# Feed-forward layers in five token tiles of 464 instead of six of 384

## The reference

```python
# attention with a bias that a small network makes from log distances
x = (log1p(|i-j|) / log1p(max(i,1)))[..., None]
bias = relu(x @ w1 + b1) @ w2                      # one value per head, i, j
attn = softmax(q @ k.T / 8 + bias);  x = attn @ v  # (2304, 512)
# first feed-forward layer ("cosine layer"), 512 -> 2048 -> 512
h = x @ w_in;  x = (h * cos(h)) @ w_out
# second ("gated layer"), 512 -> 1536 -> 512, after an RMS norm
xn = x / sqrt(mean(x*x) + 1e-6) * rms_g
out = (silu(xn @ w_gate) * (xn @ w_val)) @ w_out
```

## Time and profile before

| | |
|---|---|
| median of 3 runs | 1193.43 us (1193.26 to 1194.7) |
| profiled execution | 1196.07 us, span 1194.3 us |
| matmuls in all | 7464, of which 3 x 1632 = 4896 in the two layers |
| cosine layer, a tile | about 67.6 us |
| gated layer, a tile | about 75.0 us |

### The profile page before, as it was taken

The page is one execution under the profiler, slowest core; times in us unless marked ns, Lnnn a source line. Parts: engine busy times, 40 slices in busy tenths (PEclk is TensorE's granted clock), DMA queues, the critical chain, the costliest instruction groups (busy, mean ns, idle before and its releaser), DMA issues.

```text
span 1194.3 us, 21751 instructions
## 1 busy us (share of the span) xinstructions
PE 1164.8 (98%) x7464; PEld 1081.5 (91%) x7464; DVE 661.0 (55%) x1554; ACT 492.9 (41%) x1032; POOL 479.1 (40%) x506
## 2 busy tenths in 40 slices
PE   5879999999999999999999999999999999999998
PEld 2367777777799999999999999999999999999998
DVE  7968888888889857566575786652020020200201
ACT  7867787787833433333333333111111111111211
POOL 0057777777775433424252353851111111111111
PEclk9989999999999999999999999999999999999999
DMA  6844435352134000000000010430000000000000
GB/s 196 261 155 129 160 103 169 101 190 77 62 109 130 19 1 1 0 0 0 0 0 0 0 46 25 132 90 28 1 1 26 0 26 0 0 26 0 26 0 27
DMA packets 46680, 69.10 MB, mean 58 GB/s; under 512 B 3856, under 2 KB 27568, under 8 KB 46640
## 3 DMA queue, kind: packets, MB, share of 16 engines
q1 hardware_dynamic: 46640, 68.61, 18.5%
HBM read 53.26 MB, written 15.34 MB: 57 GB/s over the span
## 4 chain that ended last, share of the span: by engine, by line
PE 61%; issue 28%; POOL 5%; DMA 2%; ACT 2%; DVE 1%; SPq 0%; ACTq 0%; POOLq 0%; DVEq 0%
PE banks L533 7%; PE banks L859 7%; PE banks L861 7%; PE banks L860 7%; PE bank L859 6%; PE bank L861 6%; PE bank L860 6%; PE bank L575 6%; PE bank L559 5%; POOL product_low L1471 5%; PE bank L581 2%; DMA bias_scratch<-bias_stage 1%; PE bias_ps L273 1%; ACT bias_stage L191 1%; PE bank L555 1%
## 5 line engine op out<-in xcount | busy, mean ns | idle before, releaser
L859 PE MATMUL banks<-x_high,w_high_rest 128*128 128x384 f32 x672 | 225.3, 335 | 0.0
L861 PE MATMUL banks<-x_high,w_low_rest 128*128 128x384 f32 x672 | 224.5, 334 | 0.0
L860 PE MATMUL banks<-x_low,w_high_rest 128*128 128x384 f32 x672 | 224.5, 334 | 0.0
L1471 POOL TENSOR_TENSOR product_low<-X,product_high 128x384 fp32r<-128x384 f32 x72 | 72.9, 1013 | 345.2 <-ACT product_high L1414 345.2
L1452 DVE TENSOR_TENSOR X<-X,banks 128x384 f32<-128x384 f32 x72 | 39.8, 552 | 298.6 <-PE banks L861 298.6
L1254 POOL TENSOR_TENSOR product_low<-g,product_high 128x384 fp32r<-128x384 f32 x96 | 103.7, 1081 | 221.5 <-ACT product_high L1127 221.3
L859 PE MATMUL bank<-product_high,w_high_rest 128*128 128x384 f32 x480 | 160.6, 335 | 0.4 <-POOL product_low L1254 0.4
L861 PE MATMUL bank<-product_high,w_low_rest 128*128 128x384 f32 x480 | 160.4, 334 | 0.0
L860 PE MATMUL bank<-product_low,w_high_rest 128*128 128x384 f32 x480 | 160.3, 334 | 0.0
L680 DVE CUSTOM_DVE_ANT_0 probs<-banks,bias 128x576 f32<-128x576 f32 (+1 forms) x160 | 119.7, 748 | 19.5 <-PE banks L533 11.3
L628 ACT ACTIVATE probs<-probs,by_row 128x576 f32<-128x576 f32 (+1 forms) x160 | 123.3, 771 | 9.3 <-DVE by_row L680 8.3
(11 more groups left out here) (118 smaller groups left out, 2518.8 us busy)
## 6 DMA issues: line engine op xcount, KB each, us to landing
raw_qk<-in_qk SPq DMA_DIRECT2D x32, 576.0 KB, 3.8
bias_scratch<-bias_stage SPq DMA_DIRECT2D x36, 288.0 KB, 3.1
bias<-bias_scratch SPq DMA_DIRECT2D x32, 288.0 KB, 3.5
w_raw<-in_w_out SPq DMA_DIRECT2D x28, 256.0 KB, 2.6
values<-in_v SPq DMA_DIRECT2D x16, 320.0 KB, 4.1
w_raw<-in_w_in SPq DMA_DIRECT2D x16, 256.0 KB, 2.8
out_t<-X SPq DMA_DIRECT2D x5, 768.0 KB, 3.5
w_raw<-in_w_gate SPq DMA_DIRECT2D x12, 256.0 KB, 3.1
```

What stands on the lines that cost most here:

```text
L859: nc.tensor.matmul(out, high, x_high, start=start, stop=False)
L860: nc.tensor.matmul(out, high, x_low, start=False, stop=False)
L861: return nc.tensor.matmul(out, low, x_high, start=False, stop=stop)
L1471: pool.tensor_tensor(sl[f % 2][:, :], s, sh[f % 2][:, :].bitcast(F32), ALU.subtract).then_inc(s_split, 1)
```

## The change

The tile width `NT` becomes 464, so 2304 tokens are four tiles of 464 and one of 448 (`NT_LAST`). Every function of the layers takes the width as an argument, and the last tile is written out behind the loop on TensorE as well. The norm works on four pieces of 116 (or 112) tokens. So that the wider buffers fit, `turns`, `angle` and `g` become slices of the buffer that q and k land in, the high and low parts of a product share one buffer, the table of the bias stage lies in `X`, the norm's few words lie in `small`, and `ident` is freed after the cosine layer. In the gated layer the place of a stored tile in `X` is given by a list, and the low part of the last weight unit is made two chunks later.

```diff
-NT = 384
-TILES_T = TOK // NT
+NT = 464
+TILES_T = -(-TOK // NT)
+NT_LAST = TOK - (TILES_T - 1) * NT
...
-SUB = P
-NSUB = NT // SUB
+NSUB = 4
+SUB = NT // NSUB
...
+def widths_of(tile):
+    return tuple(NT if t < TILES_T - 1 else NT_LAST for t in (tile - 1, tile, tile + 1))
...
-    table = sb(ctx, "log_table", [P, LT], F32)
+    table = att.X[:, 0:LT]
...
-        self.ident = sb(top, "ident", [P, P], F32)
+        self.ident = sb(top, "ident", [P, P], F32, "right")
-        self.raw_qk = [sb(ctx, f"raw_qk{h}", [P, 2, S], F32) for h in range(2)]
+        self.raw_both = sb(top, "raw_qk", [P, 4 * S], F32, "right")
+        self.raw_qk = [self.raw_both[:, h * 2 * S:(h + 1) * 2 * S].rearrange("p (i s) -> p i s", i=2) for h in range(2)]
...
-            last = self.nc.tensor.transpose(self.rms_ps[:, i * SUB:(i + 1) * SUB],
-                                            self.inv_rms[:, i:i + 1].broadcast_to([SUB, P]), self.ident[:, :])
+            last = self.nc.tensor.transpose(self.rms_ps[:, i * sub:(i + 1) * sub],
+                                            self.inv_rms[0:sub, i:i + 1].broadcast_to([sub, P]), self.ident[0:sub, 0:sub])
...
+    def add_product(self, sb, ctx, i):
+        both = sb(ctx, f"product{i}", [P, 2, NT], F32R)
+        self.high.append(both[:, 0, :])
+        self.low.append(both[:, 1, :])
...
-        self.turns = sb(ctx, "turns", [P, NT], I32, "right")
-        self.angle = sb(ctx, "angle", [P, NT], F32, "right")
-        self.g = sb(ctx, "g", [P, NT], F32, "right")
+        turns, self.angle, self.g = (room[:, i * NT:(i + 1) * NT] for i in range(3))
+        self.turns = turns.bitcast(I32)
...
-            last = three_products(self.nc, out[:, 0:NT], self.weights, w, k, self.features.xh[:, k, :],
-                                  self.features.xl[:, k, :], k == 0, k == KC - 1)
+            last = three_products(self.nc, out[:, 0:n], self.weights, w, k, self.features.xh[:, k, 0:n],
+                                  self.features.xl[:, k, 0:n], k == 0, k == KC - 1)
...
-        tile(0, True)
-        with pe.Fori(1, T) as t:
-            tile(t, False)
+        tile(0, True, widths_of(0))
+        with pe.Fori(1, T - 1) as t:
+            tile(t, False, widths_of(1))
+        tile(T - 1, False, widths_of(T - 1))
...
+    homes = [min(t + 1, T - 2) for t in range(T - 1)] + [T - 1]
...
                     elif f == 11:
                         for d in range(KC):
-                            norm.scale(dve, T - 1, d)
+                            norm.scale(dve, T - 1, d, NT_LAST)
+                        weights.split_low(dve, LAST_UNIT)
...
                     for w in units(f):
-                        weights.split_low(dve, w)
+                        if w < LAST_UNIT:
+                            weights.split_low(dve, w)
```

More of the change, by code:

```diff
@@ L1072, in _, with up @@
     def _(pe):
-        def up(t, f, first):
+        def up(t, f, first, n):
             if first:
@@ L1077, in up, with down @@
                 pe.wait_ge(g_ready, t * C1 + (f + 1 - h_back[f]))
-            chunks.up(pe, h_ps[h_at[f]], 2 * f, t, f == 0).then_inc(h_ready, 1)
-        def down(t, f, first):
+            chunks.up(pe, h_ps[h_at[f]], 2 * f, t, f == 0, n).then_inc(h_ready, 1)
+        def down(t, f, first, n):
             if first:
@@ L1135, in free_of, with tile @@
             return (down_done, t * DOWNS) if f == 0 else (x1_ready, t * KC)
-        def tile(t, first, last):
+        def tile(t, first, last, widths):
+            back, n, ahead = widths
             for f in range(C1):
                 if not (first and f == 0):
-                    chunks.count_turns(act, h_ps[h_at[f]], t, f)
+                    chunks.count_turns(act, h_ps[h_at[f]], t, f, n)
                 if f == C1 - 1:
@@ L1191, in product, with tile @@
                 dve.wait_ge(g_split, t * C1 + f)
-            dve.tensor_tensor(g[:, :], angle[:, :], h_ps[h_at[f]][:, 0:NT], ALU.mult).then_inc(g_ready, 1)
-        def tile(t, first, last):
+            dve.tensor_tensor(g[:, 0:n], angle[:, 0:n], h_ps[h_at[f]][:, 0:n], ALU.mult).then_inc(g_ready, 1)
+        def tile(t, first, last, widths):
+            back, n, ahead = widths
             for f in range(C1):
@@ L1220, in tile @@
                     att.keep_mixed(dve, PAIRS - 1, 1, att.mixed_end)
[L1221 removed]
+                    product(t, f, first, n)
                 units = first_units(f) if first else [next_unit(f)] if last and next_unit(f) is not None else []
@@ L1345, in _, with up @@
     def _(pe):
-        def up(t, f, which, first):
+        def up(t, f, which, first, n):
             if first:
@@ L1352, in up, with down @@
                 pe.wait_ge(s_ready, t * C2 + (f - 1))
-            chunks.up(pe, val_ps[f % 2] if which else gate_ps, U1 + 3 * f + which, T + t, f == 0 and which == 0
-                      ).then_inc(val_ready if which else gate_ready, 1)
-        def down(t, f, first):
+            chunks.up(pe, val_ps[f % 2] if which else gate_ps, U1 + 3 * f + which, T + t, f == 0 and which == 0,
+                      n).then_inc(val_ready if which else gate_ready, 1)
+        def down(t, f, first, n):
             if first:
@@ L1371, in down, with tile @@
                 last.then_inc(down_done, 1)
-        def tile(t, first):
+        def tile(t, first, widths):
+            back, n, _ = widths
             for f in range(C2):
                 if f >= LAG2:
-                    down(t, f - LAG2, first)
+                    down(t, f - LAG2, first, n)
                 elif not first:
-                    down(t - 1, C2 - LAG2 + f, False)
+                    down(t - 1, C2 - LAG2 + f, False, back)
                 if not (first and f == 0):
-                    up(t, f, 0, first)
-                    up(t, f, 1, first)
+                    up(t, f, 0, first, n)
+                    up(t, f, 1, first, n)
                 if first and f == 6:
-                    norm.means(pe, T - 1)
+                    norm.means(pe, T - 1, NT_LAST)
                 elif first and f == 10:
-                    norm.spread(pe, T - 1)
-        tile(0, True)
-        with pe.Fori(1, T) as t:
-            tile(t, False)
+                    norm.spread(pe, T - 1, NT_LAST)
+        tile(0, True, widths_of(0))
+        with pe.Fori(1, T - 1) as t:
+            tile(t, False, widths_of(1))
+        tile(T - 1, False, widths_of(T - 1))
         for f in range(C2 - LAG2, C2):
-            down(T - 1, f, False)
+            down(T - 1, f, False, NT_LAST)
     @block.scalar
     def _(act):
-        def tile(t, first, last):
+        def tile(t, first, last, widths):
+            _, n, ahead = widths
             for f in range(C2):
@@ L1477, in tile @@
                         if 0 <= i < norm.SQUARE_STEPS:
-                            norm.square_step(pool, T - 1, i)
+                            norm.square_step(pool, T - 1, i, NT_LAST)
                     if f == 7:
-                        norm.power(pool, T - 1)
-        tile(0, True)
-        with pool.Fori(1, T) as t:
-            tile(t, False)
+                        norm.power(pool, T - 1, NT_LAST)
+        tile(0, True, NT)
+        with pool.Fori(1, T - 1) as t:
+            tile(t, False, NT)
+        tile(T - 1, False, NT_LAST)
     ctx.close()
@@ L1522, in build @@
         chunks.add_buffers(sb, top)
-        norm = Norm(nc, sb, sem_of, top, ins, X, banks, rms_ps, att.ident)
+        norm = Norm(nc, sem_of, ins, X, banks, rms_ps, att.ident, small[:, 2:])
         cos_layer_phase(nc, block, sb, sem_of, norm, features, weights, chunks, att)
```

302 lines of the change are left out of this document (158 added, 144 removed).

## The result

| kernel | median us (lowest to highest, executions) | against before, 95% interval |
|---|---|---|
| before | 1194.07 (1192.93 to 1195.12, 6) | 1 |
| after | 1198.30 (1197.58 to 1200.42, 6) | 1.0036 [1.0026, 1.0046] |
| after, measured again | 1197.91 (1196.84 to 1198.96, 10) | 1.0027 [1.0017, 1.0036] |

A forecast was written before the change was run, and what follows sets the result against it. The layers were taken to be bound by TensorE's list of matmuls. Terms of -10.9 for fewer matmuls, +0.4 for the norm and +0.1 for the end summed to -10.4 us, giving a median of 1183.0 us, range 1181.0 to 1188.0.

The forecast's parts named there:

- Fewer, wider matmuls: In the layers, 4080 matmuls instead of 4896, same columns streamed; 816 times a fixed 13.3 ns excess saved, 10.9 us.
- Grows with width: Rival: each layer matmul's excess over its columns grows with width, so the gain vanishes; 1193.9 us, chance 0.06.
- Addresses: Rival: 1760 layer matmuls whose moving rows start 64 bytes off run slower; at 13.3 ns each 1206.4 us, chance 0.07.
- New waits: Rival: DVE's splitting no longer fits behind 12 matmuls at eight tile starts, costing 3.0 us; 1186.0 us, chance 0.09.
- The norm: Means and spread on four pieces: 1.27 us a tile, 6.4 for five tiles against 6.0 for six; cost 0.4 us.
- The tile starts: Waits where tiles begin: helpers grow less than the down matmuls covering them; no change, bounds -0.5 and +0.5 us.
- the chains inside a chunk: DVE, ACT and POOL work within chunks of both layers stays covered by TensorE's matmuls; cost nothing.
- the moved low weight part: One 0.68 us DVE instruction behind four scalings, before gated tile 1: nothing, at most 0.7 us.
- attention's end: DVE and ACT split the wider first cosine tile there, some 0.6 us more beside other work; nothing, at most 0.6.
- Shared buffers and code: Shared buffers change addresses, not instructions, and the written-out last tile runs without gaps: nothing, unless addresses count.
- The program's end: Last of four copies and last store after TensorE, with 64 more columns: about 0.1 us more.
- The cosine layer's first tile: 338 matmuls take 69.9 us; some 62 DVE instructions widen by about 75 ns, DVE busy 59.3 us, 85% instead of 93%.

The follow-up runs named there:

- e2: The changed kernel with tiles still 464 but rows of `x_high`, `x_low` and `product` 480 long, all starts at multiples of 128 bytes: 1194.26 us, 0.9996 of before.
- e1: The changed kernel with `NT` back at 384, so six tiles, keeping the shared buffers and written-out last tile: 1193.92 us, 0.9996 of before.
- e5: The changed kernel with four tiles of 512 and one of 256, rows of `x_high`, `x_low` and products 512 long: 1190.01 us, 0.9957 of before.
- e6: The changed kernel with four tiles of 496 and one of 320, on rows 512 long: 1197.02 us, 1.0015 of before.
- e7: e5 with the norm's steps in the short last cosine tile one or two chunks later: 1189.03 us, 0.9949 of before.

## Why the prediction was wrong

*The step that failed* is "Fewer, wider matmuls". It took the excess over the columns as 13.3 ns for any width. At 464 it is 17.1 and at 448 it is 16.2 ns. Against the forecast this makes 3264 x (210.4 - 206.7) + 816 x (202.9 - 200.0) = 12.1 + 2.4 = 14.5 us. 816 matmuls less were to bring 10.9. In terms of the sum: the excess was 4896 x 13.6 = 66.6 us and is 3264 x 17.1 + 816 x 16.2 = 69.0, so +2.4 stands where -10.9 stood. (The 1.2 us between 14.5 - 10.9 and 2.4 are the base: starts of 384 columns lie 173.6 ns apart over all 4860, not 173.3.) With 0.2 for the norm and 0.55 less idle time, +2.4 makes 2.05 us; the layers grew by 1.9. Of the 3.8 ns that 464 columns have over 13.3, 1.0 goes with the row length, by e2, and 2.8 stay with the width; a lone burst shows 3.3.

*Why the evidence did not carry.* The argument went from two widths, 384 and 288, to a third. The reading itself was right: 133.1 ns is the mean of 311 such distances in attention. But the two widths proved nothing about a third: in bursts 320, 352, 384, 400 and 512 share 13.3 ns, and 416 to 480 do not; and a burst of 288 has 131.8, an excess of 11.8. That the two widths agreed in this kernel was, by these values, chance. The forecast had put its bounds at "fixed" and "growing with width" and called them both ends. The truth lay outside: from 13.6 to 17.1 ns the excess rose 26% for 21% more columns.

*The rivals.* "Grows with width" (209.4 ns, 1193.9 us, chance 0.06) came closest in size, but its rule is wrong, since 512 would have 17.7 ns by it and has 13.4. "Addresses" was real in part, and was what tipped "same" into "slower": with longer rows (e2) the same widths are level with before. But its mechanism was not the one described: it costs about 1 ns on the mean at 464 columns and nothing at 448, and not at the matmuls that start 64 bytes off. It cost 3.3 us in the layers, far below the 10.4 from which I let it decide; it decided because the gain it was to outweigh was not there. "New waits" did not happen: TensorE's idle time in the layers fell from 0.79 to 0.24 us. The rule "Back-to-back issue gap" of the Trainium skill's *TensorE: Matmul & The Clock Gate*, columns / 2.4 + 2.5 ns, holds to 0.2 ns for the bf16 bursts here (162.7, 195.8, 215.8) and for no float32r one; 1191.9 us by it was also too low.

*What was right.* The norm: 1.23 us a tile against 1.27. The tile starts, the chains inside a chunk, the moved low weight part and attention's end: no wait of TensorE on a layer line. Shared buffers and code: nothing (e1). The program's end: 4.65 us between the last layer matmul's start and the span's end, 4.37 before, 0.3 in place of 0.1. The cosine layer's first tile was off: DVE was to be busy for 59.3 us (85%) and is for 64.36 of 70.15 (92%). TensorE still did not wait. The groups by line in that tile name the instruction, first of before, then of after: count, busy us, mean ns.

```profile
L1180 DVE SCALAR_TENSOR_TENSOR angle<-turns,angle 128x384 f32<-128x384 int32 x13 | 13.9, 1072 | 0.4
```

```profile
L1194 DVE SCALAR_TENSOR_TENSOR raw_qk<-raw_qk 128x464 f32<-128x464 int32 x13 | 20.1, 1547 | 0.5
```

It took 475 ns more for 80 columns, where I had allowed 75. The shared buffer is not why, since e1 at 384 columns reads 1063 ns from it. The timelines of POOL and DVE show what is, first of before, then of after:

```profile
352.64 1.02 POOL L1254 TENSOR_TENSOR product_low<-g,product_high 128x384 fp32r<-128x384 f32 x1 [0.70 <-ACT product_high L1127]
352.99 1.08 DVE L1180 SCALAR_TENSOR_TENSOR angle<-turns,angle 128x384 f32<-128x384 int32 x1
```

```profile
352.01 1.19 POOL L1270 TENSOR_TENSOR product<-raw_qk,product 128x464 fp32r<-128x464 f32 x1 [2.12 <-ACT product L1139]
352.16 1.55 DVE L1194 SCALAR_TENSOR_TENSOR raw_qk<-raw_qk 128x464 f32<-128x464 int32 x1
```

Where an instruction of POOL is under way when DVE's step starts, the step ends a set time after POOL's: 0.40 to 0.42 us at 384 columns (40 cases), 0.48 to 0.50 at 464 (38 cases). Where none is, or POOL's starts just behind it, the step takes 0.55 to 0.56 and 0.62 to 0.65 us (54 and 42 cases). Two cases at 384 columns don't fit by their starts: POOL's began 0.31 us ahead, but DVE took 0.55 us, and it is POOL's that took 1.73 us. So the columns add some 80 ns. The other 390 or so are waiting: DVE used to come 0.36 us after POOL on the mean of that tile's 13, and now comes 0.14 us after it. This is read from both traces; no run moved the two apart.

*What the profile pair says.* Its spans differ by 2.5 us: 0.3 before the first matmul of the layers, 1.9 from there to the last one's start, 0.3 behind. The part before is scatter, for kernels with the same attention code reach that matmul between 323.84 (e1) and 325.82 us (after). The time in the layers repeats, 866.30 us in the second profile of the change, and against e1 (863.68) the width costs 2.6.

**What stays open** is why some widths keep an even rhythm at 13.3 ns and others don't, and what in the bursts ahead of them puts 448 and 496 into another. Reading the moving rows is shown as the resource; its inner rule is not.

## What to carry to other kernels

The time of a matmul over its columns is neither a constant nor a slope, so "fewer and wider" is worth something only once the new width itself has been measured, in a burst that reads rows in the kernel's own order, row length and alignment; here one burst shows 210 instead of 207 ns. For float32r in five tiles the full bank of 512 columns on rows of 512 was the only one of the widths tried that paid, 8.9 us of TensorE's busy time and 5 us of the kernel's, and its short last tile then needs other due times for the work that was planned against a long one. Read such a wait twice, once for its length and once for the granted clock behind it. Two widths with the same excess are no rule for a third.

## What the runs showed of the hardware

- Back-to-back float32r matmuls at 2.4 GHz cost 13.3 ns over their columns at 320 to 400, 15.0 to 16.6 at 416 to 480, and 13.3 at 496 and 512; bf16 2.5 to 2.7 at 384, 464 and 512. At the 1.2 GHz level the float32r excess was gone: 213.3 ns at 256 columns (e5), 266.7 at 320 (e6).
- Most of the float32r excess comes from reading the moving rows: broadcast 5.3 ns, every second element 0.44 ns for each element passed over or read (340.0 ns for 384 columns). A weight load of 32 columns instead of 128 changed 384 by 0.1 and 464 by 0.2 ns, but 480 by 3.2.
- Starts of a row matter, with no simple order. 384 columns: 173.3 to 173.6 ns from 0, 8, 64, 80 and 112 bytes on, 175 to 177 from 16, 32, 48, 96, 128 and 160, 178.3 from 4. 448 columns: 202.7 from 0, 200.1 from 64. 512 columns: 226.7 from 0, 228.9 from 64, 233.4 from 32. Most starts were run once, each behind another burst; 32 and 64 bytes at 384 and 512 gave the same within 0.4 ns when repeated.
- The same burst can take 220.0 or 223.5 ns a matmul (496 columns) or 202.7 or 206.6 (448), by what ran ahead of it.
- DVE's step with two operands in SBUF, started while POOL works, ends 0.40 to 0.42 us (384 columns) or 0.48 to 0.50 us (464) after POOL's instruction in 40 of 42 and 38 of 38 cases; alone it takes 0.56 and 0.64 us.
- After TensorE had idled 2.85 us in e5 its granted clock was 0.50 for 3.41 us; after 1.7 us in e6, 0.50 for 6.83 us; after 2.5 us in e7 it stayed at 1.00.
